# Dense stage of a fused attention and expert kernel: two groups of 384 tokens a batch in place of three of 256, with the halves of the up product in three banks in turn

## What is computed

```python
# attention, per batch b, head h, token t
cur = np.einsum('bhd,bhe->bhde', u[None] * kt, vt)
y[:, :, t] = np.einsum('bhd,bhde->bhe', rt, state + cur)
state = wt[:, :, :, None] * state + np.einsum('bhd,bhe->bhde', kt, vt)
# dense: n_tokens, d_model, d_ff = 3072, 384, 1024
a = x @ w1
b = x @ w2
h = a * b @ w3
x = h @ w_out
# experts: E = 8, F = 1024
logits = x @ w_gate
noisy_logits = logits + np.log1p(np.exp(x @ w_noise)) * noise
# the two largest per token, weights by softmax over the two
h = np.maximum(x[mask] @ w1[e], 0.0)
out[mask] += top2_w[mask, k, None] * (h @ w2[e])
```

## Time and profile before

| | |
|---|---|
| median of three runs | 1050.72 us |
| the profiled execution, its own time | 1052.72 us |
| its span | 1051.0 us |
| dense stage beside attention | about 107 to 456 us of the span |
| dense stage of the last batch | 461 to 542 us |
| TensorE busy, share of the span | 96% |
| VectorE busy, share of the span | 67% |
| ScalarE busy, share of the span | 56% |

### The profile page before, as it was taken

The page is one execution under the profiler, slowest core; times in us unless marked ns, Lnnn a source line. Parts: engine busy times, 40 slices in busy tenths (PEclk is TensorE's granted clock), DMA queues, the critical chain, the costliest instruction groups (busy, mean ns, idle before and its releaser), DMA issues.

```text
span 1051.0 us, 20538 instructions
## 1 busy us (share of the span) xinstructions
PE 1012.4 (96%) x7769; PEld 952.1 (91%) x7769; DVE 705.0 (67%) x1339; ACT 584.8 (56%) x1126; POOL 218.3 (21%) x210
## 2 busy tenths in 40 slices
PE   6999999989999899999998999999999999999995
PEld 5666899978999899999997999999999999999995
DVE  5887768666788687735685667575765857576570
ACT  4666445536555456533563566575665756566471
POOL 0000000110110110111324232433333234333421
PEclk9999999998999999999999999999999999999998
DMA  9655332333343422130757879787888978788851
GB/s 258 151 155 154 77 80 67 72 89 75 77 93 83 109 55 50 43 73 31 242 129 111 260 202 298 210 256 222 247 251 217 299 210 249 243 227 267 226 158 16
DMA packets 190887, 166.42 MB, mean 158 GB/s; under 512 B 118258, under 2 KB 174452, under 8 KB 190788
## 3 DMA queue, kind: packets, MB, share of 16 engines
q1 hardware_dynamic: 177012, 144.76, 48.2%
q0 software_dynamic: 12976, 20.32, 9.7%
q10 hardware_dynamic: 800, 0.02, 0.0%
HBM read 141.21 MB, written 25.22 MB: 158 GB/s over the span
## 4 chain that ended last, share of the span: by engine, by line
PE 86%; DMA 4%; DVE 3%; issue 2%; another core or an unknown queue 1%; POOL 1%; ACT 1%; SPq 1%; POOLq 0%; DVEq 0%; ACTq 0%
PE bank L807 19%; PE bank L1220 17%; PE pp L1236 17%; PE fx L823 5%; PE bank L823 5%; PE tr L162 3%; PE yu L1279 3%; PE yu L223 2%; PE pp L177 2%; PE fx L699 2%; PE bank L699 2%; PE yu L217 2%; PE tr L1199 2%; DMA xr<-ffn_out,who 2%; PE yu L1261 1%
## 5 line engine op out<-in xcount | busy, mean ns | idle before, releaser
L807 PE MATMUL bank<-xh,w12h 128*128 128x256 f32 x576 | 168.0, 292 | 0.6 <-DVE xl L483 0.6
L807 PE MATMUL bank<-xl,w12h 128*128 128x256 f32 x576 | 163.6, 284 | 0.8 <-issue 0.7
L807 PE MATMUL bank<-xh,w12l 128*128 128x256 f32 x576 | 163.5, 284 | 0.0
L1130 POOL DMA_INDIRECT result<-x2s,who x55 | 92.5, 1681 | 289.7 <-ACT x2s L1353 277.7
L1340 DVE SCALAR_TENSOR_TENSOR abl<-bank,abh 128x512 fp32r<-128x512 f32 x96 | 66.2, 690 | 111.7 <-ACT abh L1335 107.4
L985 POOL DMA_INDIRECT slot_entry<-entry,slot_i x48 | 48.5, 1010 | 381.1 <-DVE token_f L974 369.9
L807 PEld LDWEIGHTS bank<-xh,w12h 128*128 128x128 f32 x576 | 110.9, 193 | 3.3 <-issue 1.4
L807 PEld LDWEIGHTS bank<-xh,w12l 128*128 128x128 f32 x576 | 110.9, 193 | 1.0 <-issue 1.0
L807 PEld LDWEIGHTS bank<-xl,w12h 128*128 128x128 f32 x576 | 111.1, 193 | 0.0
L1220 PE MATMUL bank<-xh,set_up_h 128*128 128x256 f32 x384 | 109.2, 284 | 0.0
L1220 PE MATMUL bank<-xh,set_up_l 128*128 128x256 f32 x384 | 108.6, 283 | 0.0
(11 more groups left out here) (249 smaller groups left out, 2752.1 us busy)
## 6 DMA issues: line engine op xcount, KB each, us to landing
up_raw<-in_moe_w SPq DMA_DIRECT2D x93, 512.0 KB
down_raw<-in_moe_w SPq DMA_DIRECT2D x124, 384.0 KB
padded<-in_w SPq DMA_DIRECT2D x32, 144.0 KB, 2.8
padded<-in_k SPq DMA_DIRECT2D x32, 144.0 KB, 2.8
padded<-in_r SPq DMA_DIRECT2D x32, 144.0 KB, 2.9
vs<-in_v SPq DMA_DIRECT2D x32, 144.0 KB, 2.9
attention_out<-yt SPq DMA_DIRECT2D x64, 72.0 KB, 1.9
xr<-attention_out SPq DMA_DIRECT2D x12, 384.0 KB, 3.4
```

The costliest lines, as they stand in the source:

```text
L807: last = nc.tensor.matmul(bank[f % 2][:, m * TG:(m + 1) * TG], wp[:, m, kk, f * P:(f + 1) * P], xp[:, kk, :], start=(n == 0), stop=(n == 3 ...
L1130: nc.gpsimd.indirect_dma_start(out, bass.IndirectOffsetOnAxis(who[v % 4][:, s, 0:1], 0), yo[v % 2][:, s, 0:DM], None, bounds_check=N - 1, ...
```

## The change

The up product runs on 384 tokens at a time. A group has 16 half steps, a and b apart, each 9 matmuls of 384 columns in a bank of its own, and the halves go through bank 0, bank 1 and `fx` in turn. Half step n waits for what was in its bank three halves before. The down product has 9 steps, three for each of three times 128 tokens. There are 8 groups, and the tokens and the output of a group have one buffer each, so a group load waits for the split of the group before, and the copy of a group's first sum waits for the store of the group before. Each scatter step has 6 scatters. In the last batch the splits of the first visit's weights move from the down steps of the second of three groups and the up steps of the third to the up steps of the second of two, and on SP the store of the last batch's first group moves behind the loads of the first visit. The expert stage keeps its shapes; the buffers of visit 0 and 1 lie in the two token halves of the new buffer, and both gathers wait for the last split.

```diff
-TG = 256
+TG = 384
+HALVES = 2
-LENGTH = {"up": 8, "down": 6, "turn": 0, "route": 0, "place": 0,
+LENGTH = {"up": 6, "down": 6, "turn": 0, "route": 0, "place": 0,
-        xr = [sb("xr0", [P, ST, DM])]
+        tokens = sb("tokens", [P, 2 * TT * DM])
...
+            half_bank = (bank[0], bank[1], fx)
+            sum_at = (bank[1], fx, bank[1])
...
             def sp_group_load(sp, b, q):
-                if q < 2:
-                    sp.wait_ge(y_stored[q], 32 * HP * (b + 1))
-                if not (isinstance(b, int) and b == 0):
-                    sp.wait_ge(turn_free, 2 * (NG * (b - 1) + q) + 2)
-                sp.dma_start(tokens_of(q), xa[:, bass.ds(b * S + q * TG, TG)].rearrange("(k p) t -> p k t", p=P)
+                sp.wait_ge(y_stored[q], 32 * HP * (b + 1))
+                need(sp, turn_free, 2 * (NG * b + q))
+                sp.dma_start(turned_in, xa[:, bass.ds(b * S + q * TG, TG)].rearrange("(k p) t -> p k t", p=P)
...
-            def pe_up(pe, b, q, f):
+            def pe_up(pe, b, q, n):
+                f, m = divmod(n, HALVES)
-                need(pe, ab_free, KF * i + f - 1)
-                for m in range(2):
+                elif n == 1:
+                    need(pe, sum_free, sums_before(b, q, 0))
+                elif n >= 3:
+                    pe.wait_ge((a_ready, ab_free)[(n - 3) % HALVES], KF * i + (n - 3) // HALVES + 1)
...
+                        last = nc.tensor.matmul(half_bank[n % 3][:, 0:TG], wp[:, m, kk, f * P:(f + 1) * P], xp[:, kk, :],
...
             def act_down(act, b, q, part):
-                    need(act, x2_stored[q], 16 * b)
+                    if q:
+                        act.wait_ge(x2_stored[q - 1], 16 * (b + 1))
+                    else:
+                        need(act, x2_stored[NG - 1], 16 * b)
...
-            ROUTE_AT = (2, 4, 5, 6)
-            TURN_AT = 2
+            ROUTE_AT = (4, 8, 10, 12)
+            TURN_AT = 4
...
-                elif kind == "down" and q == 1 and 1 <= n <= 4:
-                    finale.append(("split", 0, n - 1))
-                elif kind == "up" and q == 2 and n in (1, 3, 5):
-                    finale.append(("split", 0, 4 + n // 2))
-                elif kind == "down" and q == 2:
-                    finale.append(("tokens", 0, 0) if n == 0 else ("split", 1, n - 1))
+                elif kind == "up" and q == 1 and n >= 4 and n % 2 == 0:
+                    finale.append(("split", 0, n // 2 - 2))
+                elif kind == "down" and q == 1:
+                    if n == 0:
+                        finale.append(("split", 0, 6))
+                    elif n == 1:
+                        finale.append(("tokens", 0, 0))
+                    elif 3 <= n < 8:
+                        finale.append(("split", 1, n - 3))
...
-                sp_group_store(sp, B - 1, 0)
                 sp_rows(sp, 0)
                 sp_weights(sp, 0)
                 for v in range(1, EARLY):
                     sp_rows(sp, v)
+                sp_group_store(sp, B - 1, 0)
+                sp_weights(sp, 1)
                 sp_group_store(sp, B - 1, 1)
-                sp_weights(sp, 1)
-                sp_group_store(sp, B - 1, 2)
```

More of the change, by code:

```diff
@@ L24 @@
 T2 = 256
+TT = T2 // P
 EARLY, BIG, SMALL = 4, 20, 7
@@ L476, in act_turn @@
             two = slice(*TURN[part])
-            nc.scalar.copy(xh[:, two, :], tokens_of(q)[:, two, :]).then_inc(xh_ready, 1)
+            nc.scalar.copy(xh[:, two, :], turned_in[:, two, :]).then_inc(xh_ready, 1)
         def dve_turn(dve, b, q, part):
@@ L708, in program @@
             psb, psem = tools(ph)
[L709 to L712, removed]
+            work = psb("work", [P, 5, TG])
+            a_sb = [work[:, i, :] for i in range(2)]
+            ab = [work[:, 2 + i, :] for i in range(3)]
+            flat_work = work[:, :, :].rearrange("p a t -> p (a t)")
             abh, abl = psb("abh", [P, KF, TG], f32r), psb("abl", [P, KF, TG], f32r)
-            x2s = [psb(f"x2s{i}", [P, ST, WA]) for i in range(NG)]
+            x2s_all = psb("x2s", [P, 2 * TT * WA])
+            x2s = x2s_all[:, 0:ST * WA].rearrange("p (s d) -> p s d", s=ST)
             noise_all = psb("noise_all", [P, NT, E])
@@ L816, in pe_down @@
                 s, third = divmod(part, 3)
-                if third == 0 and s == 0:
-                    need(pe, fx_free, fx_down(b, q, s))
+                if part == 0:
+                    pe.wait_ge(ab_free, KF * (i + 1) - 1)
+                if third == 0 and s == 2:
+                    pe.wait_ge(sum_free, sums_before(b, q, 1))
                 for f in range(3 * third, min(3 * third + 3, KF)):
@@ L825, in pe_down @@
                 if third == 2:
-                    last.then_inc(fx_full, 1)
+                    last.then_inc(sum_full, 1)
             def pe_place(pe, b, q):
@@ L921, in dve_route @@
                                                  ALU.mult))
-                    then(nc.vector.tensor_tensor(noisy[:, :, :], rest[:, :, :], x2s[q][:, :, DM:DM + E], ALU.add))
+                    then(nc.vector.tensor_tensor(noisy[:, :, :], rest[:, :, :], x2s[:, :, DM:DM + E], ALU.add))
                     other = spread(noisy[:, :, :], (E, ST), (0, E), (1, E))
@@ L996, in group_steps @@
                 for q in range(NG):
[L997 to L1001 removed]
+                    for n in range(UPS):
+                        steps.append(("up", q, n))
+                        if n in ROUTE_AT:
+                            steps.append(("route", q - 1, ROUTE_AT.index(n)))
+                    for part in range(DOWNS):
                         steps.append(("down", q, part))
[L1003 to L1004 removed]
                         if part == 2:
@@ L1043, in program @@
             sxh, sxl = (x[:, KF * P:(KF + KD) * P].rearrange("p (k t) -> p k t", k=KD) for x in (flat_wah, flat_wal))
-            hs = ab_all[:, :, :].rearrange("p a t -> p (a t)")
-            who = [psb(f"who{i}", [P, ST, 2], i32) for i in range(4)]
+            hs = flat_work[:, 0:F2]
+            who = [psb(f"who{i}", [P, TT, 2], i32) for i in range(4)]
             piece_loaded = [psem(f"piece_loaded{n}") for n in range(7)]
```

175 lines of the change are left out of this document (86 added, 89 removed).

## The result

The changed kernel takes 1054.96 us, the median of 13 runs (1051.21 to 1059.94). The kernel before took 1050.50 beside it (13 runs, 1047.40 to 1054.32). The ratio is 1.0045, with a 95% interval from 1.0027 to 1.0063: slower by 0.45%, 4.7 us by the ratio and 4.5 between these medians, where the prediction had 6.3 us less. The profiled execution took 1052.65 us, with a span of 1050.9; that of before had 1052.72 and 1051.0. So these two are equal. Within each of them much is not.

The account below looks back on a forecast made before the run. TensorE, busy 1012.4 of 1051.0 us, was taken as the bound. Terms -7.5 - 1.4 + 0.6 + 1.0 + 1.0 gave -6.3 us: 1046.4 like for like, 1044.4 us as the median; range 1034 to 1056.

Parts of the forecast that it names:

- Half steps: Up product's bank rotation: ScalarE and VectorE have two halves, 3.1 us, where they had 2.16 us; no cost.
- Last batch: First expert weights and their splits: ScalarE waits 0 to 3 us against 3.1 us of cover; +1.0 us (0 to 5).
- Up product: Dense stage: 1152 matmuls of 384 columns at 173.3 ns, 199.7 us in place of 207.2; -7.5 us.
- Place and first group: Four fewer place steps on TensorE, -1.4 us; first up step waits for a larger token split, +0.6 us (0 to 1.0).
- Second scores: Attention: second score step waits for the first's mask with one half step between, in six groups; +1.0 us.
- The start of the expert stage: Scatters before the expert visits begin earlier but are more; 0.
- Stops: TensorE stops where group stores meet scatters: two kept, 12 us for both, so 0; ends -12 and +18.
- the last batch stalls: Rival: loads or VectorE's splits come later than the cover, at up to 6 us: 1050 us; chance 0.08.

Follow-up runs that it names:

- splits later: Changed kernel with only the last batch's weight splits moved to later half steps and down steps: 1056.03 us, ratio 1.0054 to the kernel before.
- all three edits: Changed kernel with visit 2 and 3 gathers before the last group's scatters, weight splits later, three routing passes behind products: 1031.58 us (0.9794); again 1026.02 us (0.9815).
- before with its gathers first: Kernel before with the gathers of visits 2 and 3 issued ahead of the last group's scatters: 1040.12 us, ratio 0.9869.
- routing behind products: Changed kernel with three routing passes moved from half steps 8, 10, 12 to 9, 11, 13, behind a product: 1047.03 us, ratio 0.9985.
- the two experiments on them: Changed kernel with gather, split and routing edits, plus group stores issued later: 1033.37 us; or plus five groups' entries written to consecutive rows: 1024.07 us, time not compared.
- gathers first: Changed kernel with the gathers of visits 2 and 3 issued ahead of the very last group's scatters: 1044.84 us, ratio 0.9935 to the kernel before.

## Why the prediction was wrong

**Half steps, "No cost": the step that failed, by 9.4 us.** The 3.1 us of cover was right. What VectorE has ahead of the product in its queue was not counted: 0.95 + 0.95 + 2.1 us. By the up runs it cost 7.5 us beside the attention and, together with the splits, 2.9 in the last group; it cost 9.4 by the medians, which take both in, and 8.9 in the changed kernel itself. Put into the sum, 9.4 us turn -6.3 into +3.1, which lies within the measured interval of 2.8 to 6.6 us. For the last batch I had named VectorE's load, for the other batches not. The distance in steps is no cover until the work queued between is taken off.

**Last batch, +1.0 (0 to 5): under-sized.** ScalarE's turn came at 48.3 us after the batch's start (448.4), 2.4 later than I had it; the weights had landed only at 53.2. They went out at 49.6 (498.05), not at 45 to 46: I had taken some 4 us off because the batch's first store no longer stood ahead, and in before it had not held them up either (its scatters landed last, at 498.0, with who behind them at 499.05). And the loads' own landing, 3.54 us, was not in the sum. Where nothing behind it takes it up this costs 6.0 us; in the changed kernel the edit of the splits alone was worth nothing, since the chain of landings began 4.1 us earlier there but took 3.3 us longer.

**Up product, -7.5: right.** 173.3 ns from matmul to matmul; a last-batch group takes 25.0 us from first up to first down matmul (448.4 to 473.3), as forecast. The Trainium skill (TensorE: Matmul & The Clock Gate, Back-to-back issue gap) has a formula for the isolated gap that comes to 162.5 ns at this width, an estimate; the measurement disagrees here as it did at 256 columns.

**Place and first group: right as far as it was read.** The wait before the first up step grew from 0.60 to 1.26 us, for the +0.6; the -1.4 of place steps was not read by itself. **Second scores, +1.0: too high.** Neither in the changed kernel nor with all three edits is there a wait over 0.3 us before scores in the attention stages.

These terms add up. Up product, place and first group are -8.3 us, and all three edits against before with its gathers first measured -8.5. With 9.4 for the routing and 6.0 for the splits that makes +6.9, and the two kernels with only the gathers mended differ by some 7 us, by ratios from two rounds. So the stream was forecast rightly, and what failed are two waits that the sum had at 0 and at +1.0. In the kernels as they were the chain hides part of the second.

**"The start of the expert stage: 0; its scatters begin earlier but are more": near right as a difference, by luck.** I had not followed the chain of landings behind GpSimd's queue. It took 34.1 us before (542.18 to 576.29) and 44.6 after, for two more scatters twice, 14 us of landing in place of 12, and 14.4 us of gather in place of 10.7 (from its first issue); and it began 12.2 us earlier. It costs the changed kernel 11.0 us and before 13.9, so it explains none of the slowdown. That it can swallow a lead shows in one pair: with the splits later TensorE was 5.6 us ahead and the tokens came 0.8 us earlier. With routing behind products 3.8 of 4.6 us got through.

**Stops, 0 (two kept): wrong in kind.** By the two experiments on them they go with the scatters, not with a store that meets them, and they vary: 6.36 and 2.85 us in one trace of before, 2.34 in the other, none over 1.5 in two of the changed kernel.

The rival "the last batch stalls" (0.08, 1050 us) named one of the two places, the weights. None named VectorE's routing beside the attention, nor GpSimd's chain.

What stays open: between the profiled executions the change costs nothing to 2.4 us, between the medians 4.5 and 6.3. The changed kernel's other runs took 2 to 3 us more in the median than its profiled ones and no trace shows where. Nor is it known why the chain's length differs from one execution to the next, or why engines go without signals behind scattered writes.

## What to carry to other kernels

Cover counted in steps is to be reduced by the work that stands ahead in the same queue, on every engine and in every stage; moving such work by one step was worth more here than the change itself. When a wait turns up, mend it in the kernel before as well and compare the mended pair: a large wait that both kernels share explains no difference between them, though it can hide what an edit upstream is worth. Take a second trace before you price a wait: the same place had 4.6 us of idle in one execution and 10.4 in the next. And follow the chains that do not pass through the busiest engine (writes, their landing, the gather queued behind them) to the place where it meets them: here their order alone was worth 11 to 14 us.

## What the runs showed of the hardware

128 entries of 8 bytes written by a direct transfer to consecutive rows landed in 3.1 us (median of 30). Six indirect writes to scattered rows took 9.12 us to land behind the last of them where neither store nor weights met them (486.64, changed kernel), and 14.44 us where they did (533.84, splits later); four of them took 11.5 us in before. The Trainium skill (DMA: Bandwidth & Descriptors, Anatomy of one DMA) fits a transfer at about 2.0 us plus its bytes over 436 GB/s, most of it the wait until the write is confirmed; the consecutive write took some 1 us more than this estimate, the scattered ones several times as long.

A group's store of 576 KB landed in 3.0 us where it met no scatters and in 13 to 14 where it did (274.14 and 391.11, all three edits).

In every trace with scattered writes some group's scatters were followed, mostly 3 to 9 us after the last issue, by a stretch of 1.5 to 6.5 us without any signal between engines, most of them nearly without packets. TensorE stopped in some of them, where it needed a signal, and went on in others. With a stop of 5.02 us went 6.83 us at a granted clock of 0.50, with one of 5.07 in another kernel (gathers first) 3.41, with one of 14.84 us 17.07.
